# First products of a fused attention and expert kernel: products nobody reads at the start, one load on another queue, three-operand forms, and a regrouped end of the first expert's rows

## The chip, the cores and the metric

The kernel runs on one core of one Trainium2 chip, in one launch. The metric is the device time of that launch in microseconds (us), the median of three runs. The engines are TensorE (PE; its weight loads are shown apart as PEld), VectorE (DVE), ScalarE (ACT), GpSimd (POOL) and SyncE (SP), which here only issues DMAs.

## The reference, cut to what matters

```python
# attention: B=2, H=8, S=576, D=64; causal window of 128 keys, a linear bias per head
scores = where(mask, q @ k.T / 8 + bias[head], -1e9); attn = softmax(scores); x = attn @ v
x = x.transpose(0, 2, 1, 3).reshape(1152, 512)            # 1152 tokens, 512 wide
# experts: E=8, F=1024, capacity 288; each token goes to its best expert
logits = x @ w_gate; e = argmax(logits); gate = softmax(logits)[e]
disp[e, count[e]] = x[i]                                   # in order of the tokens, up to the capacity
y = relu(disp @ w1) @ w2; out[i] = gate[i] * y[e, pos[i]]
# then a dense layer, 512 -> 2048 -> 512, with h * sigmoid(h) between
```

## The kernel before

**Attention.** The 1152 tokens are 10 blocks (`NTOK`) of 128 rows; blocks 4 and 9 have 64. For each block t the loop at L1204 to L1241 gives PE this order: scores of the first four heads, the transposes of the probabilities, the turn of x of block t-2 with its logits, the values, the transpose of q of block t+1 (`turn(..., qraw)`), scores of the other four heads, transposes of their probabilities, the transpose of k of block t+1, and the values. DVE adds the bias and finds the minimum (L795), ACT takes the exponentials (L613) and copies q and k out of PSUM (`take_q`, `take_k`, L596 and L602). SP loads q, k and v of every block, in that order, by `load_qkv` (L330).

**Routing.** DVE finds each block's best expert (`first_match`), its places (`place_found`) and gate, and POOL multiplies x by the gate (L538) and scatters the rows to `dispatch_dram` (`scatter`, L518). For the last three blocks (t = 7, 8, 9, from `LAST`) ACT multiplies by the gate (`gate_x`, L675). The scattered rows of the seven blocks before them come back by one load (`load_first_slots(0)`, L362); PE brings them into the first expert's columns by products with the identity (L1270). The rows of the last three blocks do not wait for memory: POOL builds a 0/1 matrix of the slots (`select_first`, L524 to L529), and PE multiplies by it (`selected`, L1195), adding into the same four banks, `FIRST_X`. The turn of each bank c of the four is: two products with the identity, then the one product of block 9. ACT (L692) and DVE (L1008) take the bank as a high and a low part, `xT`.

**Experts.** PE goes through eight experts, most used first. Each is eight steps `up` of one F chunk, four steps `turn` that transpose the next expert's rows (`turn_slots`, L1284 to L1287), and four steps `down`. The first `turn` waits for `xd_in` and, because the second expert's width 200 is over `FIRST` = 192, for `xd_rest` too (L1326 to L1328). These come from SP, in this order (L399 to L415): it waits for the plan that DVE makes at L962 to L981 (`plan_ready`), loads the second expert's `w1` (four pieces of 512 KB), waits for the scatters of all blocks, loads the other slots of expert 0, waits for PE's `step_done`, loads the next expert's first slots, waits until the other slots of expert 0 have landed (L368), and loads the next expert's other slots. Behind them comes `w2`.

**Weights.** Every weight is split into a high part (a copy to fp32r, `w_hi`) and a low part (`w_lo`, the difference, written over the raw one). For the first expert there are eight pieces. POOL makes the high part of piece t in block t (`high_here`) and its low part in block t+1 (`low_here`), for `EARLY` = 6 pieces; ACT makes the last two high parts behind its last `gate_x` (L686 to L688).

## Time and profile before

| | us |
|---|---|
| median of 3 runs | 460.9 (460.63 to 463.35) |
| the profiled execution, its own time | 460.6 |
| its span, from the first to the last instruction | 458.8 |
| PE busy in the span | 439.1 (96%) |
| POOL busy | 240.3 (52%) |
| DVE busy | 229.1 (50%) |
| ACT busy | 221.0 (48%) |
| share of PE in the chain that ended last | 82% |

So 1.8 us of the launch lie outside the span, and the profiled execution is 0.3 us under the median. The page's slices show PE at 90% or more in nearly all of them. The granted clock of TensorE is given as a share of its full speed; the mean over the span is 0.991.

### The profile page before, as it was taken

To read this page: it belongs to the slowest core of one execution; us is meant where nothing else is said; L and a number is where in the kernel's file an instruction comes from. 1 tells how busy PE (TensorE), PEld (TensorE's weight loads), DVE (VectorE), ACT (ScalarE), POOL (GpSimd) and SP (SyncE) were. 2 spreads that over 40 slices of the span, in tenths; PEclk is the share of its full clock that TensorE was granted. 3 is DMA by queue.
4 is the path that set the end of the run, shared out by engine and by line. 5 is a ranking of instruction groups with operands and counts; after the bars stand their busy time and mean duration, and the time that the engine had idled before them with its cause. 6 is when DMAs were issued, how large, how long until landed. Compare 5 with 4: busy or idle time off the path is not lost.

```text
span 458.8 us, 8374 instructions
## 1 busy us (share of the span) xinstructions
PE 439.1 (96%) x2917; PEld 397.0 (87%) x2917; DVE 229.1 (50%) x732; ACT 221.0 (48%) x549; POOL 240.3 (52%) x172
## 2 busy tenths in 40 slices
PE   5999999899999999999999999999999999999993
PEld 4687778679999999999999999998999989999982
DVE  4478588878475775865854552222222231322230
ACT  4777778645576556656677643131212222221230
POOL 4005888856979989999999987502000002000002
PEclk9999999998999999999999999999999999999997
DMA  9999970038987767786887400001000001000002
GB/s 180 268 289 270 280 209 14 24 114 300 367 279 278 251 221 244 290 301 239 267 299 241 164 1 1 0 3 67 2 0 0 0 0 69 0 0 0 0 0 74
DMA packets 54568, 64.29 MB, mean 140 GB/s; under 512 B 32096, under 2 KB 32096, under 8 KB 54528
## 3 DMA queue, kind: packets, MB, share of 16 engines
q1 hardware_dynamic: 52752, 59.08, 41.6%
q0 software_dynamic: 1776, 4.73, 2.8%
q8 instruction: 20, 0.33, 0.3%
q14 instruction: 20, 0.16, 0.1%
HBM read 54.35 MB, written 9.44 MB: 139 GB/s over the span
## 4 chain that ended last, share of the span: by engine, by line
PE 82%; DVE 7%; ACT 7%; issue 2%; DMA 1%; POOL 1%; POOLq 0%; DVEq 0%
PE bank L1280 15%; PE bank L1281 14%; PE bank L1282 14%; PE bank L1302 14%; PE bank L1301 7%; PE bank L1121 4%; PE bank L1138 3%; DVE w_lo L1038 3%; PE bank L1299 3%; PE bank L1172 2%; PE bank L1160 2%; ACT prob L613 2%; PE bank L1105 2%; ACT w_hi L643 2%; PE bank L1300 1%
## 5 line engine op out<-in xcount | busy, mean ns | idle before, releaser
L490 POOL TENSOR_TENSOR w_lo<-w_raw,w_hi 128x1024 fp32r<-128x1024 f32 x72 | 179.2, 2520 | 16.1 <-ACT w_hi L643 14.5
L1072 DVE TENSOR_TENSOR g_full<-bank,sigmoid 128x384 f32<-128x384 f32 x48 | 26.8, 558 | 130.0 <-ACT sigmoid L730 124.8
L584 POOL DMA_INDIRECT out_dram<-out_stage,permcol x9 | 8.8, 973 | 150.8 <-ACT out_stage L750 147.5
L730 ACT ACTIVATE sigmoid<-bank 128x384 f32<-128x384 f32 x48 | 23.6, 492 | 125.4 <-PE bank L1282 116.6
L643 ACT ACTIVATE w_hi<-w_raw 128x1024 fp32r<-128x1024 f32 x74 | 77.8, 1053 | 0.0
L1003 DVE TENSOR_REDUCE bank<-bank 128x192 f32<-128x384 f32 (+5 forms) x96 | 49.0, 512 | 38.7 <-PE bank L1302 38.7
L1280 PE MATMUL bank<-x_hi,w_hi 128*128 x192 | 65.0, 338 | 0.0
L1282 PE MATMUL bank<-x_hi,w_lo 128*128 x192 | 64.6, 336 | 0.0
L1281 PE MATMUL bank<-x_lo,w_hi 128*128 x192 | 64.4, 336 | 0.0
L1302 PE MATMUL bank<-hidden,w_hi 128*128 128x384 f32 (+5 forms) x224 | 63.0, 351 | 0.0
L1280 PE MATMUL bank<-w_hi,g_hi 128*128 128x512 f32 x144 | 56.9, 395 | 0.8 <-DVE g_lo L1076 0.8
L1302 PE MATMUL bank<-xT,w_hi 128*128 128x384 f32 (+5 forms) x192 | 57.4, 354 | 0.0
L1281 PE MATMUL bank<-w_lo,g_hi 128*128 128x512 f32 x144 | 56.5, 392 | 0.0
L1301 PE MATMUL bank<-hidden,w_lo 128*128 128x192 f32 (+5 forms) x224 | 55.6, 248 | 0.7 <-DVE hidden L1018 0.6
L1282 PE MATMUL bank<-w_hi,g_lo 128*128 128x512 f32 x144 | 56.1, 389 | 0.0
L1301 PE MATMUL bank<-xT,w_lo 128*128 128x192 f32 (+5 forms) x192 | 48.8, 254 | 0.0
L613 ACT ACTIVATE prob<-prob,neg_max 128x256 f32<-128x256 f32 (+2 forms) x80 | 37.3, 469 | 19.8 <-DVE neg_max L795 19.7
L1301 PEld LDWEIGHTS bank<-hidden,w_lo 128*128 128x128 f32 x224 | 42.7, 190 | 2.0 <-DVE hidden L1018 1.9
L1302 PEld LDWEIGHTS bank<-hidden,w_hi 128*128 128x128 f32 x224 | 42.2, 188 | 0.0
L1280 PEld LDWEIGHTS bank<-x_hi,w_hi 128*128 128x128 f32 x192 | 36.1, 188 | 1.7 <-issue 0.2
L1281 PEld LDWEIGHTS bank<-x_lo,w_hi 128*128 128x128 f32 x192 | 36.0, 188 | 1.5
L1301 PEld LDWEIGHTS bank<-xT,w_lo 128*128 128x128 f32 x192 | 37.1, 193 | 0.0
(146 smaller groups left out, 792.1 us busy)
## 6 DMA issues: line engine op xcount, KB each, us to landing
w_raw<-in_moe_w_dram SPq DMA_DIRECT2D x64, 512.0 KB, 5.9
dispatch_dram<-zeros SPq DMA_DIRECT2D x4, 1152.0 KB, 8.0
w_raw<-in_moe_w_in_dram SPq DMA_DIRECT2D x8, 512.0 KB, 5.0
w_raw<-in_moe_w_out_dram SPq DMA_DIRECT2D x8, 512.0 KB, 6.1
dispatched<-dispatch_dram SPq DMA_DIRECT2D x9, 384.0 KB, 7.6
q_raw<-in_q_dram SPq DMA_DIRECT2D x8, 256.0 KB, 5.5
k_raw<-in_k_dram SPq DMA_DIRECT2D x8, 256.0 KB, 5.8
v_raw<-in_v_dram SPq DMA_DIRECT2D x8, 256.0 KB, 5.9
```

The source lines that it names most:

```text
L490: nc.gpsimd.tensor_tensor(wlo[s][:, sl], raw[s][:, sl], whi[s][:, sl], ALU.subtract).then_inc(pool_lo, 1)
L613: nc.scalar.activation(prob[0:r, u % 2, m, c0:c0 + n], prob[0:r, u % 2, m, c0:c0 + n], ACT.Exp, bias=nmin[0:r, t % 2, h:h + 1], scale=-1.0 ...
L643: nc.scalar.activation(whi[s][:, sl], raw[s][:, sl], ACT.Copy).then_inc(whi_ready, 1)
L730: nc.scalar.activation(sig[:, f % 2, :], bank[f % 4][:, 0:TB], ACT.Sigmoid).then_inc(sig_ready, 1)
L1003: nc.vector.tensor_reduce(bk[:, 0:w], both, axis=AX.X, op=ALU.add).then_inc(summed, 1)
L1072: nc.vector.tensor_tensor(gf[:, f % 2, :], bank[f % 4][:, 0:TB], sig[:, f % 2, :], ALU.mult).then_inc(gf_ready, 1)
L1121: last = nc.tensor.matmul(bS[u % 2][hh][0:r, j * 2 * P + c0:j * 2 * P + c0 + n], qT[d, t % 2, hp, 0:r], kT[d, hp, k0:k0 + n], start=True, ...
L1280: nc.tensor.matmul(dst, ah, bh, start=first, stop=False)
L1281: nc.tensor.matmul(dst, ah, bl, start=False, stop=False)
L1282: return nc.tensor.matmul(dst, al, bh, start=False, stop=last)
L1301: nc.tensor.matmul(dst, al, x[:, 0, 0:w], start=False, stop=False)
L1302: return nc.tensor.matmul(both, ah, x[:, :, 0:w], start=False, stop=last)
```

## The change

1. PE multiplies the identity by itself five times (`WAKE`) into a bank of the probabilities before its first transpose. Nobody reads the result.
2. The load of k of block 0 is issued by ACT, as its first instruction, and no longer by SP between q and v.
3. `EARLY` falls from 6 to 5: POOL makes one high part (in block 5) and one low part (in block 6) fewer, ACT makes three high parts instead of two, the first two of them earlier, behind `take_xT(9)` and behind `gate_exp(9)`, and POOL makes two low parts behind its last scatter instead of one.
4. `sums_guarded` (L813) and the one-hot of `first_match` (L868) become three-operand instructions with a tile of zeros as the third operand.
5. The slot matrix of block 9 is made by DVE behind `slot_found(9)` and ahead of the plan, not by POOL. POOL's three last scatters wait for `last_slots` instead. Two memsets at the start zero the rows that block 9 lacks, and `selected` takes 128 rows for it instead of 64.
6. PE brings the rows from memory into all four banks first, then multiplies block 9's rows into all four.

```diff
-    EARLY = 6
+    EARLY = 5
+    WAKE = 5
@@ SP, load_qkv
+                    if t == 0 and src is k:
+                        continue
@@ POOL
+            nc.gpsimd.memset(xg[:, NTOK - 1, :], 0.0)
+            nc.gpsimd.memset(sel[:, NTOK - 1 - LAST, :], 0.0)
...
-            for t in range(LAST, NTOK):
+            for t in range(LAST, NTOK - 1):
                 select_first(t)
             pool.wait_ge(xd_in, 16)
+            pool.wait_ge(last_slots, NTOK - LAST)
             for t in range(LAST, NTOK):
                 scatter(t)
             pool.wait_ge(plan_ready, 2)
-            low_here(1, EARLY - PIECES, EARLY + 1)
+            for n in range(EARLY, POOLED):
+                low_here(1, n - PIECES, n + 1)
@@ ACT
+            act.dma_start(kraw[0:ROWS[0], 0, :].rearrange("p (h d) -> p h d", h=H),
+                          k[0, :, 0:ROWS[0], :].rearrange("h p d -> p h d")).then_inc(k_in[0], 16)
...
             take_xT(NTOK - 1)
+            act.wait_ge(pool_lo, EARLY)
+            weight_high(1, EARLY - PIECES, 16)
             gate_x(NTOK - 2)
             gate_exp(NTOK - 1)
+            weight_high(1, EARLY + 1 - PIECES, 16)
             gate_x(NTOK - 1)
-            act.wait_ge(pool_lo, EARLY)
-            for p in range(EARLY, SPLITS):
+            for p in range(EARLY + 2, SPLITS):
                 weight_high(1, p - PIECES, 16)
@@ DVE
-                start(nc.vector.tensor_scalar_add(rsum1[0:r, :], rsum[0:r, t % 3, :], 1e-9))
+                start(nc.vector.scalar_tensor_tensor(rsum1[0:r, :], rsum[0:r, t % 3, :], 1e-9, zeros[0:r, 0:H], ALU.add, ALU.add))
...
-                nc.vector.tensor_scalar(onehot[0:r, t, :], wdesc[0:r, :], best[0:r, at_t], None, ALU.is_equal).then_inc(onehot_ready, 1)
+                nc.vector.scalar_tensor_tensor(onehot[0:r, t, :], wdesc[0:r, :], best[0:r, at_t], zeros[0:r, 0:E],
+                                               ALU.is_equal, ALU.add).then_inc(onehot_ready, 1)
...
             slot_found(NTOK - 1)
+            r = ROWS[-1]
+            dve.wait_ge(last_slots, NTOK - LAST)
+            nc.vector.tensor_scalar(sel[0:r, NTOK - 1 - LAST, :], slot_no[0:r, :], place[0:r, NTOK - 1:], sbase[0:r, NTOK - 1:],
+                                    ALU.subtract, ALU.is_equal).then_inc(last_sel, 1)
@@ PE
-                return nc.tensor.matmul(FIRST_X[c][:, 0:FIRST], xg[0:r, t, c * P:(c + 1) * P], sel[0:r, t - LAST, :],
+                return nc.tensor.matmul(FIRST_X[c][:, 0:FIRST], xg[:, t, c * P:(c + 1) * P], sel[:, t - LAST, :],
...
             pe.wait_ge(ident_ready, 1)
+            for _ in range(WAKE):
+                nc.tensor.matmul(bP[0][:, 0:P], ident[:], ident[:], start=True, stop=True)
...
-                if c == 0:
-                    pe.wait_ge(sel_ready, 3)
-                    pe.wait_ge(gated, NTOK)
+            pe.wait_ge(last_sel, 1)
+            pe.wait_ge(gated, NTOK)
+            for c in range(KC):
                 selected(NTOK - 1, c, False, True).then_inc(step_done, 1)
```

## Rows read from the trace of the kernel before

**Rows 1.** The timeline of PE in the first 22 us: start, duration, instructions, idle before.
```profile
4.20 1.09 PE L1105 MATMUL bank<-ident,q_raw 128*128 128x128 f32 x4 [4.20 <-DMA q_raw<-in_q_dram]
...
7.08 1.22 PE L1121 MATMUL bank<-kT,qT 64*128 64x128 f32 x8 [0.69 <-ACT kT L602]
...
13.09 2.08 PE L1121 MATMUL bank<-kT,qT 64*128 64x256 f32 x8 [0.69 <-ACT kT L602]
...
17.02 0.65 PE L1105 MATMUL bank<-ident,q_raw 128*128 128x128 f32 x4
17.60 1.13 PE L1121 MATMUL bank<-kT,qT 64*128 64x256 f32 x8
```

**Rows 2.** The timeline of all engines at the start: identity, k, ACT's exponentials.
```profile
1.24 0.29 POOL L458 TENSOR_SCALAR_AFFINE_SELECT ident<-ident 128x128 f32<-128x128 f32 x1 [0.24 <-POOL ident L461]
...
5.28 0.71 PEld L1105 LDWEIGHTS bank<-ident,k_raw 128*128 128x128 f32 x4 [0.39 <-DMA k_raw<-in_k_dram]
...
11.58 0.19 ACT L613 ACTIVATION_READ_ACCUMULATOR prob<-prob,neg_max 128x1 f32 x1
```

**Rows 3.** The chain that ended last, its first piece: start, duration, what.
```profile
0.79 3.27 DMA q_raw<-in_q_dram
```

**Rows 4.** DVE beside POOL late in the attention (timeline of both engines).
```profile
85.55 2.35 POOL L490 TENSOR_TENSOR w_lo<-w_raw,w_hi 128x1024 fp32r<-128x1024 f32 x1
...
87.18 0.76 DVE L813 TENSOR_SCALAR row_sum<-row_sum 128x8 f32<-128x8 f32 x1
```

**Rows 5.** Lines L813 and L868: duration ns min/median/max, first and last start.
```profile
L813 DVE TENSOR_SCALAR row_sum<-row_sum x10: 152/161/760, 22.8 to 92.9; 128x8 f32<-128x8 f32 x8, 64x8 f32<-64x8 f32 x2
...
L868 DVE TENSOR_SCALAR onehot<-wdesc,best x10: 223/231/306, 26.7 to 95.2; 128x8 fp32r<-128x8 f32 x8, 64x8 fp32r<-64x8 f32 x2
```

**Rows 6.** The timeline where the first expert's rows are built (all engines).
```profile
94.17 0.72 ACT L675 ACTIVATE x_gated<-x_tile,gate 128x512 f32<-128x512 f32 x1 [1.42 <-DVE gate L897]
...
96.11 1.55 PE L1198 MATMUL bank<-selection,x_gated 128*128 128x192 f32 x8
...
96.81 0.72 ACT L675 ACTIVATE x_gated<-x_tile,gate 64x512 f32<-64x512 f32 x1 [1.63 <-DVE gate L897]
...
97.27 0.15 DVE L965 TENSOR_SCALAR values<-bank 128x8 f32<-128x8 f32 x1
...
97.49 0.58 PE L1270 MATMUL bank<-ident,dispatched 96*128 96x96 f32 x4
98.50 0.59 PE L1198 MATMUL bank<-selection,x_gated 64*128 64x192 f32 x2 [0.43 <-POOL selection L528]
...
102.67 0.69 PE L1299 MATMUL bank<-xT,w_hi 128*128 128x384 f32 x1
```

**Rows 7.** DVE's bias instructions at the start (timeline): eight of 256 columns.
```profile
2.96 2.84 DVE L902 TENSOR_SCALAR bias<-rel 128x256 f32<-128x256 f32 x8 [2.96 <-POOL rel L458]
```

**Rows 8.** Windows of 1 us: length, busy of each engine, granted clock, DMA share, GB/s.
```profile
103.00:104.00 1.00, 1.00 (x5) 1.00 (x5) 0.36 (x1) 0.11 (x1) 1.00 (x1) 0.50 0.70 246
...
106.00:107.00 1.00, 1.00 (x9) 1.00 (x9) 0.83 (x6) 0.00 (x0) 0.00 (x0) 1.00 1.03 422
```

**Rows 9.** SP's issues in the timeline, behind the plan.
```profile
101.40 1.94 SPq L340 DMA_DIRECT2D w_raw<-in_moe_w_dram  x4
105.80 0.35 SPq L370 DMA_DIRECT2D dispatched<-dispatch_dram  x1
...
111.03 0.33 SPq L370 DMA_DIRECT2D dispatched<-dispatch_dram  x1
```

**Rows 10.** The tile view of `dispatched`: time to landing of L370's issues at 105.80 and 111.03.
```profile
DMA to landing us min/median/max: 5.1/5.1/5.1
...
DMA to landing us min/median/max: 2.4/2.4/2.4
```

**Rows 11.** The chain where `up` ends and `turn` begins: start, duration, what.
```profile
113.44 0.12 issue
113.56 1.18 PE bank L1286 x12
```

More of the change, by code:

```diff
@@ L211, in build @@
         gate_ready, gated, slot_ready, dve_step = sem("gate_ready"), sem("gated"), sem("slot_ready"), sem("dve_step")
-        last_slots, sel_ready = sem("last_slots"), sem("sel_ready")
+        last_slots, sel_ready, last_sel = sem("last_slots"), sem("sel_ready"), sem("last_sel")
         rest_turned, rest_high, rest_parts = sem("rest_turned"), sem("rest_high"), sem("rest_parts")
@@ L1195, in selected @@
             def selected(t, c, first, last):
-                r = ROWS[t]
-                return nc.tensor.matmul(FIRST_X[c][:, 0:FIRST], xg[0:r, t, c * P:(c + 1) * P], sel[0:r, t - LAST, :],
+                return nc.tensor.matmul(FIRST_X[c][:, 0:FIRST], xg[:, t, c * P:(c + 1) * P], sel[:, t - LAST, :],
                                         start=first, stop=last)
             pe.wait_ge(ident_ready, 1)
+            for _ in range(WAKE):
+                nc.tensor.matmul(bP[0][:, 0:P], ident[:], ident[:], start=True, stop=True)
             turn(0, qraw, q_in, bX)
```

## The prediction

> **What bounds the kernel now.** I read the page first: PE is busy for 96% of the span and holds 82% of the chain that ended last, so a change pays where it shortens PE's stream or a wait that PE ends up sitting in. From the slices and windows I took two stretches that the diff touches: the start, and the 95th to 115th us, where the attention hands over to the experts. In the timeline of PE at the start the reader should see that equal work takes different times: four transposes 1.09 us at 4.20 and 0.65 at 17.02, eight score products of 256 columns 2.08 at 13.09 and 1.13 at 17.60 [rows 1]. So PE ran at the lower of its clocks up to about 17 us, though the windows print a granted clock of 1.00 there (no change of clock is on record before it). The second such stretch is on record: 0.50 at 103 us (1.2 GHz), 1.00 again from 106 (2.4 GHz) [rows 8]. Third, the chain and SP's issues around 113 us: the first `turn` begins at 113.56, 0.12 us after the last `up` product gave way [rows 11], and the load it needs, issued at 111.03, took 2.4 us, to 113.43 [rows 9, 10]. The waits view names a DVE instruction for PE's stop of 0.3 us there, but that one had long been done; `turn` waits for three semaphores, and only the load fits. PE's stream and this load therefore end within 0.2 us of each other. That decides most of what follows.
>
> **The five products at the start.** The identity is ready at about 1.55 and q lands at 4.06 [rows 2, 3]. One 128-column transpose is 0.27 us at the low clock; a full fp32 product of the same columns is issued as two such records, as the scores are, so it costs at most 0.55 us and, by start to start, about 0.43. Five make 2.2 us (2.7 at worst) from 1.6: done at 3.8, or 4.3 at worst, so they cost 0 to 0.2 us. They do no work; what they can buy is the clock. If PE is at the high clock from the first scores at 7.08, those end 0.6 us earlier (half of 1.22), and so do the exponentials behind them. Then ACT is next: it was free of its exponentials at 11.77 [rows 2] and then waited for PE's transposes of k; 0.6 earlier that is 11.2, with 0.6 for the copy of k the scores of block 1 start at 11.8 instead of 13.09: 1.3 us. From there to the scores at 17.60 PE has 4.5 us of work at the low clock that take about 2.7 at the high one (2.08 to 1.1, and transposes, values and transposes of q at 0.6, 0.5 and 0.6): another 1.8. Together 3.1 us, and everything behind it moves with it, because the attention is one chain of PE, DVE and ACT, and the loads of w1, w2 and the plan follow that chain. Low end 0 (the clock does not come earlier), high end 3.5 (it is high for the first transposes too).
>
> Does the clock rise? In the trace it stayed low through three us of transposes and 128-column scores from 7.08 on, with one gap of 0.7, and rose only after 13.09 to 17, when PE had no gap and long scores [rows 1]. With the five products PE is at work from 1.6 to 6.4 with one gap of under 1 us, which it never was there. I take it as somewhat likelier than not. The Trainium skill (TensorE: Matmul & The Clock Gate, Part 4: PE-mode transpose) says that transposes do not count as PE activity for the clock; the trace is in line with it, as the rise followed the scores, but it cannot part it from the gaps. By that rule the five products would be the first work that counts, and the sum would be the 3.1 to 3.5 us; with transposes counting alike it would be nearer 0 to 3.
>
> **k on ACT's queue.** k moves ahead by one issue and then shares the DMA engines with q. Before, q landed at 4.06 and PE's weight load waited 0.39 us for k until 5.28 [rows 2, 3]. Both together should be there by 4.7: q's transposes start up to 0.6 later, k's no longer wait. At the low clock that is a loss of up to 0.6 (4.7 + 2.2 = 6.9 against 6.4), at the high clock a gain of 0.4 (4.7 + 1.3 = 6.0). If the queues do not disturb each other, it is 0. I take 0, as the forecast's clock lies between the two. ACT's issue is hidden: it has nothing to do before the copy of q. The Trainium skill (DMA: Bandwidth & Descriptors, Issuing engines are not separate DMA queues) speaks against a gain: such loads interleave on the same engines, and only the issuer's time is saved. By it the sum would carry the +0.6 where the clock stays low.
>
> **The three-operand forms.** Ten of each. L813 has a median of 161 ns and L868, with a rounded output, 231 [rows 5]; the nearest three-operand times lie between, so each may cost 0 to 0.08 us. Only those of the blocks where DVE ends the chain count, about four of twenty: 0 to +0.3. What they may save: L813 took 0.76 us at 87.18, until POOL's low part of 85.55 ended [rows 4], one more was long. The work behind both waits for ACT's copy of x anyway, which ended later, so the 0.6 us hide. Value +0.1, bounds −0.3 to +0.3.
>
> **POOL's and ACT's pieces.** POOL loses a high part (1.06) and the low part at 85.55 (2.35) in the attention; scatter 6 leaves 1.5 us earlier, but PE took its rows at 97.49 straight behind block 8's products (96.11 and 1.55), so it did not wait for them [rows 6]. ACT's added high parts take 1.05 us each and go into its idle 1.42 and 1.63 us ahead of `gate_x` [rows 6]; behind them wait the two `gate_x` and PE's products. That cover is thin: if `gate` comes earlier by more than 0.4, ACT ends it. POOL's second late low part (2.4 us) ends near 106, and the first `down` asks behind `turn`, at 114.7 [rows 11]. All 0.
>
> **The regrouped rows.** Before, from 97.49 to 102.67, 5.2 us [rows 6]: 0.43 waiting for POOL's matrix, then product and selection in turn. After: four product groups of 0.58 and four selections that with 128 rows take 1.55 together, as block 8's did: 3.9 us, ready at 101.4. Gain 1.2 us at PE. With it PE is denser, so that the low clock of 102 to 105.5, which costs half of 3.4, may not come: another 1.7. `up` would end 1.2 or 2.9 us earlier than 113.44.
>
> **But the first `turn` waits for the load.** Its chain is plan, w1 (101.40), the other slots of expert 0 (105.80, 5.1 us behind the 2 MB of w1), then the next expert's (111.03, 2.4) [rows 9, 10]. Nothing PE gains enters it. What does: DVE's matrix for block 9 stands ahead of the plan. The bias instructions cost 0.35 each for 256 columns [rows 7]; 192 columns and the wait for `slot_i` give 0.4 (0.3 to 0.5; never the 1.0 of POOL). Queued behind: the plan, excess, SP's w1 and so the load. Against it, POOL's scatters start 1.1 us earlier and leave the DMA engines to w1 sooner, worth 0 to 0.5. Net +0.2 (−0.2 to +0.5). So the 1.2 to 2.9 us become idle time of PE ahead of `turn`.
>
> **Sum.** Profiled span 458.8: start −3.1 taken at −2.7, as the clock may come a little later than the first scores, k 0, forms +0.1, regrouping 0, plan +0.2: 456.4. With the 1.8 us outside the span and 0.3 from the profiled time to the median: 458.5.
>
> **The rivals.**
> A, the forecast, 0.45: start pays, handover is swallowed: 458.5, own range 457.4 to 459.8.
> B, 0.30, ends slower: the clock does not rise before the 13th us. Then only the costs are left: k +0.6, forms +0.1, plan +0.2, and 461.8. The point from which it decides: the four transposes at about 5 us and the scores at 13 us keep 1.09 and 2.08. For it: the record of 7 to 12 us above.
> C, 0.13: the load isn't the bound, because w1 with no scatter beside it lands over 1 us earlier; then 1.2 to 2.9 of the handover count: with the middle, 2.0, 456.5 with A, 459.8 with B. Against it: four pieces of w1 already ran back to back.
> D, 0.07: the clock falls behind 106 instead, since PE idles ahead of `turn`; 1.7 us at PE are lost where nothing hides them: 460.2 with A, 463.5 with B.
> E, 0.05: the change does nothing: 460.9.
>
> **Range and chances.** The ends are C at its full 2.9 with A, rounded down for a high start (455.3), and B with the upper bounds of plan and forms (+0.5 more: 462.3); B with D and the corners left out hold about 0.1. Within 1% is 456.3 to 465.5, about what a measurement can tell from no change. Faster than that needs C with A and most of its gain: 0.1. Slower needs B, D and more: 0.03.
>
> **What would show it.** A: transposes near 0.6 us at 5 to 8 us, the scores of block 1 at about 11.5 to 12, the first `up` near 98.7 (101.5 minus the shift), and an idle PE of 1 to 3 us ahead of the first L1286. B: long scores at 13 us. C: no such idle time, L1286 over 5 us earlier than 113.56. D: a granted clock of 0.50 behind 110. My forecast fails if PE doesn't wait ahead of `turn`, or if the first 17 us keep their length.

## The result and the profile after

| | before | after |
|---|---|---|
| median of 17 runs each, us | 461.9 (460.63 to 471.70) | 464.4 (461.98 to 476.46) |
| ratio of the times, 95% interval | | 1.0048 [1.0028, 1.0068] |
| profiled execution, its own time, us | 460.6 | 467.3 |
| its span, us | 458.8 | 465.6 |
| its mean granted clock | 0.991 | 0.977 |
| first product of the first expert, us | 102.67 | 104.72 |
| first `turn`, us | 113.56 | 117.83 |
| first `up` product of the second expert, us | 123.78 | 130.55 |
| first product of the dense layer, us | 249.87 | 256.88 |

Ratios and means here and below leave out the executions more than 1.5% above the fastest of the same kernel; medians are over all. The changed kernel is 0.5% slower, 464.4 us where 458.5 was forecast and 462.3 was the upper end. Before itself came out 1.0 us higher in 17 runs than in the three shown ahead; against the three alone, 460.9, the ratio makes 463.1, still above the range. The profiled execution of after is one of its longer ones (467.3 with a median of 464.4) and ran at the lowest mean clock of them (0.977; the mean of the 14 is 0.988), so the places of its losses count here, not their sum.

The timeline of PE in the changed kernel, first 22 us, to be laid beside [rows 1]:

```profile
1.57 2.50 PE L1218 MATMUL bank<-ident 128*128 128x128 f32 x10 [1.57 <-POOL ident L461]
4.62 1.11 PE L1121 MATMUL bank<-ident,q_raw 128*128 128x128 f32 x4 [0.54 <-DMA q_raw<-in_q_dram]
5.53 1.06 PE L1121 MATMUL bank<-ident,k_raw 128*128 128x128 f32 x4
7.27 1.22 PE L1137 MATMUL bank<-kT,qT 64*128 64x128 f32 x8 [0.69 <-ACT kT L609]
...
13.28 2.08 PE L1137 MATMUL bank<-kT,qT 64*128 64x256 f32 x8 [0.69 <-ACT kT L609]
...
17.38 0.66 PE L1121 MATMUL bank<-ident,q_raw 128*128 128x128 f32 x4
17.97 1.13 PE L1137 MATMUL bank<-kT,qT 64*128 64x256 f32 x8
```

The five products (ten records) fill 1.57 to 4.07, and the clock takes no notice: transposes 1.11 us, block 1's scores 2.08, the short forms only from 17.38. q's transposes start at 4.62 for 4.20, k's no longer wait, the first scores start at 7.27 for 7.08. That is rival B's sign.

The windows of the changed kernel at the handover (stretch in us, its length, then busy time and instructions of PE, PEld, DVE, ACT, POOL; granted clock, DMA share, GB/s):

```profile
106.00:111.00 5.00, 5.00 (x37) 5.00 (x36) 4.79 (x8) 0.00 (x0) 3.52 (x2) 1.00 0.99 395
111.00:114.00 3.00, 3.00 (x22) 2.87 (x20) 2.86 (x10) 1.53 (x4) 0.17 (x1) 1.00 0.92 236
114.00:115.00 1.00, 0.12 (x1) 0.00 (x0) 1.00 (x3) 1.00 (x2) 1.00 (x1) 1.00 0.06 18
115.00:116.00 1.00, 0.00 (x0) 0.00 (x0) 1.00 (x4) 0.47 (x2) 1.00 (x1) 1.00 0.04 14
116.00:117.00 1.00, 0.00 (x0) 0.00 (x0) 1.00 (x4) 0.71 (x2) 1.00 (x2) 0.66 0.85 211
117.00:120.00 3.00, 2.17 (x13) 2.20 (x14) 2.53 (x8) 2.98 (x8) 3.00 (x2) 0.50 0.93 315
120.00:123.00 3.00, 3.00 (x12) 3.00 (x12) 0.54 (x2) 0.36 (x2) 3.00 (x2) 0.50 1.02 377
123.00:126.00 3.00, 3.00 (x22) 3.00 (x22) 0.83 (x2) 1.28 (x2) 1.06 (x2) 0.97 1.03 417
```

PE is busy without a break to 114.1, then idle to 117.83, and in that idle time, at about 116.3, the granted clock falls to 0.50 (1.2 GHz), where it stays until 123.2. From 120 to 123 PE is fully busy and gets through 12 instructions, from 123 to 126 through 22. Before had its short low stretch ahead of this, from 102.1 to 105.5 [rows 8], and none behind it before the last microseconds of the span. The same profiled execution also ran at 0.50 from 89.0 to 99.3, 10.2 us where before had 3.4; with it the first expert starts 2.05 us later although the regrouped rows took less.

The chain that ended last in the changed kernel, between 103 and 120 us (start, duration, what), and SP's DMA issues there (start, duration of the issue):

```profile
103.82 3.60 DMA dispatch_dram<-x_gated,slot_i
...
107.44 7.66 DMA dispatched<-dispatch_dram
...
115.25 2.45 DMA dispatched<-dispatch_dram
117.70 0.14 issue
117.83 2.15 PE bank L1303 x12
```
```profile
104.37 1.93 SPq L343 DMA_DIRECT2D w_raw<-in_moe_w_dram  x4
107.44 0.35 SPq L373 DMA_DIRECT2D dispatched<-dispatch_dram  x1
108.06 0.34 SPq L365 DMA_DIRECT2D dispatched<-dispatch_dram  x1
115.25 0.33 SPq L373 DMA_DIRECT2D dispatched<-dispatch_dram  x1
```

It is the chain of [rows 9 to 11] with two differences. All of it is 3.0 us later here (w1 at 104.37 for 101.40). And the other slots of expert 0 took 7.7 us to land instead of 5.1 [rows 10], so the load that the first `turn` waits for went out 10.9 us behind w1, not 9.6.

### The profile page after: what moved, and what is told of

It reads as the page before. It is cut to its first block, busy times and chain, and to the rows that moved or that the text cites. A ratio compares the mean times of both kernels' runs of the same rounds, so it can differ in the third digit from the quotient of the medians.

```text
span 465.6 us, 8394 instructions
## 1 busy us (share of the span) xinstructions
PE 445.0 (96%) x2927; PEld 404.0 (87%) x2927; DVE 230.4 (49%) x733; ACT 222.0 (48%) x550; POOL 238.8 (51%) x172
## 4 chain that ended last, share of the span: by engine, by line
PE 77%; ACT 8%; DVE 8%; DMA 4%; issue 2%; POOL 0%; POOLq 0%; SPq 0%
PE bank L1297 14%; PE bank L1298 14%; PE bank L1299 14%; PE bank L1319 12%; PE bank L1318 6%; PE bank L1137 4%; DVE w_lo L1054 3%; PE bank L1154 3%; PE bank L1176 3%; PE bank L1188 2%; ACT prob L620 2%; DMA dispatched<-dispatch_dram 2%; ACT w_hi L650 2%; PE bank L1316 2%; PE bank L1121 2%
## 5 line engine op out<-in xcount | busy, mean ns | idle before, releaser
L650 ACT ACTIVATE w_hi<-w_raw 128x1024 fp32r<-128x1024 f32 x75 | 78.9, 1053 | 0.0
L1319 PE MATMUL bank<-hidden,w_hi 128*128 128x384 f32 (+5 forms) x224 | 64.3, 356 | 0.0
```

The lines of the kernel that those rows point to most:

```text
L650: nc.scalar.activation(whi[s][:, sl], raw[s][:, sl], ACT.Copy).then_inc(whi_ready, 1)
L1319: return nc.tensor.matmul(both, ah, x[:, :, 0:w], start=False, stop=last)
```

## The experiments

Each kernel ran with runs of before on the same chip; before had medians of 461.4 to 462.7 us in the sessions, and single runs behind its means from 459.2 to 465.9 us. "Ratio" is that of the times to before's, with its 95% interval. "Mean" is the kernel's mean time, beside 461.8 to 462.2 for before; "clock" is its mean granted clock, 0.989 to 0.991 for before.

| kernel | median us | ratio [95%] | mean us | clock |
|---|---|---|---|---|
| p_start | 461.6 | 1.0003 [0.9976, 1.0031] | 461.8 | 0.990 |
| p_early | 462.0 | 1.0019 [0.9989, 1.0049] | 462.5 | 0.988 |
| p_forms | 461.7 | 1.0006 [0.9977, 1.0035] | 462.1 | 0.988 |
| p_rows | 465.8 | 1.0095 [1.0061, 1.0129] | 465.8 | 0.982 |
| x_rows_order | 462.8 | 0.9990 [0.9956, 1.0024] | 462.7 | 0.991 |
| x_rows_keep | 462.6 | 0.9986 [0.9956, 1.0015] | 462.3 | 0.994 |
| x_after_order | 462.3 | 1.0000 [0.9976, 1.0025] | 462.4 | 0.993 |
| x_before_order | 462.5 | 0.9977 [0.9948, 1.0006] | 461.7 | 0.990 |
| x_after_keep | 463.1 | 1.0016 [0.9987, 1.0044] | 462.6 | 0.994 |
| x_after_order2 | 464.8 | 1.0051 [1.0021, 1.0080] | 464.2 | 0.988 |
| x_before_order2 | 464.6 | 1.0060 [1.0030, 1.0091] | 464.7 | 0.986 |
| x_wake12 | 463.9 | 1.0040 [1.0015, 1.0066] | 463.7 | 0.986 |
| x_after_skip | 464.2 | 1.0034 [1.0002, 1.0065] | 463.7 | 0.990 |
| x_wake12_split | 464.0 | 1.0034 [1.0011, 1.0058] | 463.7 | 0.985 |
| x_before_split | 463.3 | 1.0029 [1.0014, 1.0044] | 463.3 | 0.984 |
| x_after_skip_split | 463.2 | 0.9999 [0.9965, 1.0033] | 462.1 | 0.990 |
| x_after_skip_keep | 461.8 | 1.0006 [0.9981, 1.0031] | 462.1 | 0.994 |

### One part at a time

**p_start**: before with parts 1 and 2 only.

```diff
+                    if t == 0 and src is k:
+                        continue
@@ ACT, first instruction
+            act.dma_start(kraw[0:ROWS[0], 0, :] ...)
@@ PE
+            for _ in range(WAKE):
+                nc.tensor.matmul(bP[0][:, 0:P], ident[:], ident[:], start=True, stop=True)
```

> Only the start of the change: five unread products and block 0's k on ACT's queue. Theory H (the loss is made in the handover, by the first expert's rows): +0.3 us, the shift of the first scores from 7.08 to 7.27 that the changed kernel shows, and no more. Rival S (the start makes the loss: it costs more in other executions than in the profiled one, or shifts the blocks so that the clock falls at a worse place): +1.5 to +3 us. If the clock came up earlier in some executions, this kernel would be faster by up to 3 us.

**p_early**: part 3 only (`EARLY = 5`, ACT's two high parts moved ahead of its last `gate_x`, POOL's second late low part).

> Only EARLY = 5: one high and one low part fewer on POOL in the attention, ACT's high parts in the gaps ahead of gate_x. Theory H: 0 +- 0.5 us. Rival E (ACT's high part of 1.05 us delays gate_x, and through it PE's products and the scatter; or POOL is now the one that is late behind the last scatter): +1 to +2.5 us.

**p_forms**: part 4 only, the two three-operand forms.

> Only the three-operand forms of L813 and L868. Theory H: 0 to +0.3 us. A rival in which they wait for POOL's low parts longer than the old forms did: +1 us or more, with L813 or L868 near 0.7 us in several blocks.

**p_rows**: parts 5 and 6 only, block 9's matrix on DVE and the regrouped products.

> Only the first expert's rows: block 9's matrix by DVE ahead of the plan, 128 rows, PE takes all rows from memory first. Theory H: +1.5 to +2.5 us, nearly the whole loss; excess 0.5 us or more later behind slot_i, PE idle for 2 us or more ahead of the first turn (0.12 before), and in some executions a granted clock of 0.50 behind 110 us. Rivals S and E: 0 +- 0.5 us.

Parts 1 to 4 cannot be told from nothing. Parts 5 and 6 alone lose 3.7 us (1.0095, seven runs), more than the 1.5 to 2.5 expected and more than the full change. Their profile has the wait and the low clock, with no other part of the change in it. The line of `turn` in PE's timeline of p_rows, then its windows:

```profile
114.20 2.15 PE L1292 MATMUL bank<-ident,dispatched 96*128 96x96 f32 x12 [3.55 <-DMA dispatched<-dispatch_dram]
```
```profile
112.00:115.00 3.00, 0.80 (x5) 0.83 (x6) 1.35 (x4) 1.38 (x4) 3.00 (x2) 0.79 0.69 204
115.00:118.00 3.00, 3.00 (x17) 3.00 (x15) 1.10 (x3) 1.30 (x4) 3.00 (x2) 0.50 0.98 356
118.00:121.00 3.00, 3.00 (x15) 3.00 (x14) 0.29 (x1) 0.00 (x0) 0.07 (x1) 0.58 1.05 409
121.00:124.00 3.00, 3.00 (x23) 3.00 (x22) 1.36 (x4) 1.56 (x4) 1.24 (x1) 1.00 1.03 419
```

The rows are ready early (the first `up` at 101.25, before at 102.67), as forecast. PE then idles 3.55 us, the clock is at 0.50 from 113.7 to 120.5, `turn` comes 0.6 us later than before's, the second expert 13.2 us behind `turn` where before had 10.2. 0.6 and 3.0 make 3.6; the two profiled spans differ by 3.3 (462.1 and 458.8), the means by 3.7.

### Is it the wait, the clock, or something else?

**x_rows_order**: p_rows, with the other slots of expert 0 and both loads of the next expert's slots between the halves of w1.

```diff
-            load_w1(expert[1], 2)
+            load_w1(expert[1], 2, range(2))
             ...
+            load_w1(expert[1], 2, range(2, PIECES))
```

> p_rows with another order of SP's issues: only two pieces of the second expert's w1 ahead of the loads of the slots, the other two behind them. Theory I (the loss is PE's idle time ahead of the first turn, which waits for xd_rest behind 2 MB of w1, and the clock that falls after it): the first turn begins 2 us or more earlier than 114.2, PE is idle for under 1 us ahead of it, no granted clock of 0.50 follows, and the time is 4 to 6 us under p_rows, 0.5 to 2.5 under before. Rival J (the clock falls because of the sparse products of the whole handover, whatever the first turn waits for): the fall behind the first turn stays and the gain over p_rows is 0 to 2 us.

**x_rows_keep**: p_rows, with 14 products of the identity ahead of the first `turn`, into the bank that `turn` overwrites; nobody reads them.

```diff
+                        if c == 0 and e == 0:
+                            for _ in range(14):
+                                nc.tensor.matmul(bk[:, 0:P], ident[:], ident[:], start=True, stop=True)
```

> p_rows with 14 unread products of the identity by itself (0.22 us each at the high clock, some 3 us) ahead of the first turn. The wait for xd_rest stays as it is; only PE isn't idle in it. Theory I, its second half (the idle time makes the clock fall, and that costs more than the wait): no fall behind 110 us, first turn at about 114.2 as in p_rows, second up near 124.5 instead of 127.4, the time 2.5 to 3.5 us under p_rows and 0.5 to 1.5 over before. If the clock falls all the same, 0 to 1 us under p_rows.

**x_after_order**, **x_before_order**: the first edit on after and on before.

> The changed kernel with the same order of SP's issues as x_rows_order. Theory I: its loss of 2.5 us goes and 1 to 2 us of gain come in its place, so 0.5 to 2 us under before. Rival J: it stays at +1 to +2.5 us.

> The kernel before with the same order of SP's issues alone. PE waited 0.12 us there, so Theory I: 0 to -0.5 us. If the order is worth something by itself (w1 or w2 arriving at a better time), or costs something (w1's last pieces late for ACT), it shows here: beyond -1 or +1 us.

Both cures take the loss away: 462.7 and 462.3 for 465.8, clear of noise against p_rows. Neither brings the gain over before (0.5 to 2.5 us) that x_rows_order was expected to show. The second leaves the transfers as they are and only keeps PE at work; it raises the mean clock from 0.982 to 0.994, and 3.4 of the 3.7 us come back. So most of p_rows' price is the low clock behind the wait, not the wait. (The one profile of x_rows_keep has a span of 601 us, so only its times are used.) In x_rows_order `turn` starts at 113.80 without waiting and no low stretch follows; but the second half of w1 goes out only at 110.84, and PE then waits for it: the second expert's `up` comes at 126.28, later than before's 123.78. This order of loads has a price of its own there.

**x_after_keep**: after, with the same 14 products.

> The changed kernel with 14 unread products of the identity ahead of the first turn. If the loss of the changed kernel is what the idle time ahead of the first turn does to the clock: no granted clock of 0.50 begins within 7 us behind 110 us, the second expert's first up comes 10 us behind the first turn (12.7 in the changed kernel, 10.2 in the one before), and the time is 1.5 to 2.5 us under the changed kernel, within 0.5 us of before. If that was peculiar to p_rows: no difference to the changed kernel, +2.5 us over before.

**x_after_order2**, **x_before_order2**: as the order edit, but the second half of w1 ahead of the next expert's other slots.

```diff
-            load_w1(expert[1], 2)
+            load_w1(expert[1], 2, range(2))
             ...
-            load_dispatched(expert[1])
+            load_first_slots(expert[1])
+            load_w1(expert[1], 2, range(2, PIECES))
+            load_other_slots(expert[1])
```

> The changed kernel with w1's last two pieces issued behind the second expert's first slots and ahead of its other slots, so that they don't wait for a landing (in x_after_order they were issued at 111 us, and the down steps and the second up came late). If the handover's gain of about 1.2 us at PE is real and was only given back to loads: first turn at about 112, second up 10 us behind it, 1 to 2 us under before. If the order of the loads is not what holds it: no difference to x_after_order, 0 to +0.5 us over before.

> The kernel before with the same order of loads as x_after_order2, alone. It waited 0.12 us ahead of the first turn: 0 to -0.5 us. A gain beyond -1 us would say that executions other than the profiled one wait there for longer.

x_after_keep, PE's timeline and two of its windows:

```profile
111.24 3.29 PE L1344 MATMUL bank<-ident 128*128 128x128 f32 x28
115.27 1.18 PE L1303 MATMUL bank<-ident,dispatched 96*128 96x96 f32 x12 [0.75 <-DMA dispatched<-dispatch_dram]
```
```profile
112.00:115.00 3.00, 2.52 (x23) 2.33 (x21) 2.98 (x9) 2.17 (x5) 3.00 (x2) 1.00 0.28 85
115.00:118.00 3.00, 2.73 (x24) 2.76 (x25) 2.36 (x7) 2.54 (x8) 3.00 (x2) 1.00 0.93 317
```

The chain of loads still takes its time (the last one issued at 112.60, `turn` at 115.27), but the idle piece of PE ahead of it is 0.75 us and the clock stays at 1.00; `turn` takes 1.18 us, not 2.15, and the second expert comes 10.2 us behind it, as in before. The mean is 462.6 us, for 464.4 of the full change; the ratios, 1.0016 [0.9987, 1.0044] and 1.0048 [1.0028, 1.0068], overlap at their edges, so on the full change the cure is less certain in the times than on p_rows.

x_before_order2 was expected to change nothing (0 to −0.5 us) and missed, and so became a test from the other side: a kernel with none of the change's parts, in which one load was put behind 1 MB of w1. Its line of `turn` and its windows:

```profile
116.00 2.15 PE L1288 MATMUL bank<-ident,dispatched 96*128 96x96 f32 x12 [3.06 <-DMA dispatched<-dispatch_dram]
```
```profile
115.00:118.00 3.00, 2.00 (x13) 2.03 (x14) 1.09 (x3) 2.23 (x5) 3.00 (x3) 0.50 1.05 371
118.00:121.00 3.00, 3.00 (x13) 3.00 (x13) 0.37 (x1) 0.38 (x2) 1.86 (x1) 0.50 1.05 402
```

With the wait of 3.06 us comes the low clock (114.8 to 121.6), the second expert 12.9 us behind `turn` instead of 10.2, and 464.6 us, 1.0060 [1.0030, 1.0091]. x_after_order2 missed too, 464.8 us where up to 2 us under before were hoped for: PE waited 2.20 us, `turn` came at 116.31, and here the clock fell only 1.0 us into the work, at 117.3, until 120.7. The first edit, without the piece of w1 ahead of the load, cured after (x_after_order: `turn` at 113.42, 462.3 us) and moved before by less than can be told from nothing.

**x_after_skip**: after, where SP leaves out the other slots of expert 0 when nobody is in them (`excess` is 0 here).

```diff
-            load_other_slots(0)
+            n_over = sp.value_load(excess[0:1, 0:1], min_val=0, max_val=C)
+            with sp.If(n_over <= 0):
+                sp.sem_inc(xd_rest, 16)
+            with sp.Else():
+                load_other_slots(0)
+            loaded[0] = 1
```

> The changed kernel; SP leaves out the load of expert 0's other slots where all widths suffice (nobody reads them then), so that the second expert's other slots are issued some 4 us earlier, behind w1 and its first slots. Theory I: the first turn waits no longer for a landing that waits for a landing; it begins about 112, PE is idle under 1.5 us ahead of it, the clock doesn't fall there, and the time is 2 to 4 us under the changed kernel, 0 to 1.5 us under before. Rival: other loads land late instead and it stays over before by 1 us or more.

Its own profile, PE's line of `turn`, SP's issues, and a window:

```profile
113.91 1.18 PE L1308 MATMUL bank<-ident,dispatched 96*128 96x96 f32 x12 [2.76 <-DMA dispatched<-dispatch_dram]
```
```profile
101.75 1.87 SPq L343 DMA_DIRECT2D w_raw<-in_moe_w_dram  x4
105.54 0.33 SPq L365 DMA_DIRECT2D dispatched<-dispatch_dram  x1
106.09 0.35 SPq L373 DMA_DIRECT2D dispatched<-dispatch_dram  x1
```
```profile
115.00:118.00 3.00, 3.00 (x24) 3.00 (x23) 2.62 (x9) 2.29 (x7) 3.00 (x2) 1.00 1.06 399
```

One load less in the chain, and the load that `turn` needs goes out at 106.09, 5 us earlier than before's; yet it lands 7.7 us later, at 113.8, 12.0 us behind the 2 MB of w1 issued at 101.75, as in before (12.0; 13.3 in after). That fits w1's bytes setting when the loads behind them arrive, not their number; no run changed the bytes alone. PE's wait is still 2.76 us, where under 1.5 was expected. This execution kept its clock and took 460.9 us. The eleven runs behind the mean fall apart: four took 460.9 to 462.3 us at 0.990 to 0.995, two 463.4 and 463.8 at 0.992, five 464.6 to 467.1 at 0.984 to 0.987. The likeliest reading is that after a wait near 3 us the clock sometimes falls and sometimes does not; only one execution has a trace.

**x_after_skip_keep**: x_after_skip, with 14 unread products. The expectation places them ahead of the first `turn`; the edit placed them elsewhere, ahead of the first `up` product of the first expert.

```diff
                     if kind == "up":
                         if c == 0:
                             pe.wait_ge(pool_lo, pooled_by(e, PIECES))
+                        if c == 0 and e == 0:
+                            for _ in range(14):
+                                nc.tensor.matmul(bk[:, 0:P], ident[:], ident[:], start=True, stop=True)
```

> The changed kernel with both remedies at the first turn: SP leaves out the other slots of expert 0 when nobody is in them, and 14 products whose results are not read keep PE at work ahead of the turn. If the idle time ahead of the turn and the low clock behind it are the whole of what the changed kernel loses, this one should keep a mean clock near 0.993, show no granted clock of 0.50 behind 110 us, and take 461.0 to 462.0 us, 1 to 2 us less than skipping alone (463.7). If they are not the whole, it stays at 462.4 to 463.7, as the unread products alone did (462.6).

PE's timeline shows where they ran:

```profile
101.89 3.36 PE L1344 MATMUL bank<-ident 128*128 128x128 f32 x28 [0.85 <-issue]
114.27 1.16 PE L1308 MATMUL bank<-ident,dispatched 96*128 96x96 f32 x12
```

So this run does not fill the wait; it sends PE there 3 us later. The first `up` comes at 105.01, `turn` at 114.27 without a wait (its load had landed at 114.0), no low clock behind 110: 461.8 us, mean 462.1, 0.994, level with before, though PE carries 3.1 us of useless work. That bears out that PE's time ahead of `turn` is bounded by the load. The interval (0.9981 to 1.0031) overlaps that of x_after_skip (1.0002 to 1.0065), so the difference of 1.6 us between the two means is not clear of noise.

### Does an earlier clock at the start pay?

**x_wake12**: p_start with `WAKE = 12`.

> p_start with twelve unread products instead of five: they run from 1.6 to about 6.7 us, so q's transposes begin some 2.2 us later than the load allows. Theory F (five are too few, a longer stretch without a gap lifts the clock): the clock is at 1.0 by 8.5 us, the transposes of q of block 1 take near 0.6 us, and the gain of 3 us pays for the delay: -1.5 to +0.5 us. Theory G (unread products of this kind do not lift it, only the later stretch does): the clock rises at 11 to 17 us as before and the time is +1.5 to +2.5 us.

Twelve products do lift the clock, but the time does not come down to the range that was expected in that case (−1.5 to +0.5 us): the mean is 1.6 over before's. PE's timeline at the start:

```profile
1.58 4.72 PE L1208 MATMUL bank<-ident 128*128 128x128 f32 x24 [1.58 <-POOL ident L461]
6.14 0.60 PE L1110 MATMUL bank<-ident,q_raw 128*128 128x128 f32 x4
```

Transposes take 0.60 us from 6.14, block 1's scores start at 12.66 for 13.09 and take 1.13 for 2.08. The exponentials lead before's by 2.1 us at 21 us (21.05 for 23.16) and still at 44 (44.24 for 46.38). Then, all engines between 54 and 57 us:

```profile
54.17 2.35 POOL L493 TENSOR_TENSOR w_lo<-w_raw,w_hi 128x1024 fp32r<-128x1024 f32 x1
54.27 2.28 DVE L818 TENSOR_SCALAR row_sum<-row_sum 64x8 f32<-64x8 f32 x1
```

A DVE operation on 8 columns takes 2.28 us, until POOL's low part of 54.17 ends. Its median in before is 161 ns [rows 5]. At 62 us the lead has become a lag of 1.2 (62.29 for 61.07). The same row took 2.02 us in p_start and 2.17 in x_rows_order, whose clocks rose at 10.9 and 11.3 us. In before, whose clock rose at 16.8, two were hit, by 0.58 and 0.76 only [rows 4, 5]. The Trainium skill (SBUF — State Buffer, Who interferes with whom) says that DVE and GpSimd share a pair of ports, and that where an instruction of DVE takes that pair, whoever issues first has it for a whole instruction and the other is blocked. The trace agrees: DVE's row starts 0.10 us behind POOL's and ends at 56.55, POOL's at 56.52.

**x_wake12_split**, **x_before_split**: x_wake12 and before, each low part of the attention cut into four operations of 256 columns. **x_after_skip_split**: x_after_skip with the same cut.

```diff
-                nc.gpsimd.tensor_tensor(wlo[s][:, sl], raw[s][:, sl], whi[s][:, sl], ALU.subtract).then_inc(pool_lo, 1)
+                for n in range(cuts):
+                    w = PIECE // cuts
+                    sl = slice(part * PIECE + n * w, part * PIECE + (n + 1) * w)
+                    last = nc.gpsimd.tensor_tensor(wlo[s][:, sl], raw[s][:, sl], whi[s][:, sl], ALU.subtract)
+                last.then_inc(pool_lo, 1)
@@ the blocks of the attention
-                    low_here((t - 1) // PIECES, (t - 1) % PIECES, t)
+                    low_here((t - 1) // PIECES, (t - 1) % PIECES, t, 4)
```

> x_wake12 with POOL's low parts of the attention cut into four instructions of 256 columns. Theory K (a short DVE instruction that meets a running low part waits for its end): no L813 or L868 over 0.8 us, the blocks keep their 2 us ahead of before, and the time is 1.5 to 3 us under x_wake12. Rival L (the early gain is lost to another engine or load that paces the blocks): the short instructions are short and the time stays within 0.7 us of x_wake12.

> The kernel before with the low parts of the attention cut in the same way, alone. Theory K: executions of before that were hit by such a stall gain up to 2 us, those that were not gain nothing, so -0.3 to -1.5 us in the median and a narrower spread. Rival L: 0, or +0.5 us for the added instructions on POOL.

> The changed kernel with both, the load left out and the low parts cut. If both theories hold, it beats before by 1 to 3 us; if only I holds, it is equal to x_after_skip.

At this place the mechanism holds. The timeline of x_wake12_split:

```profile
54.22 2.78 POOL L495 TENSOR_TENSOR w_lo<-w_raw,w_hi 128x256 fp32r<-128x256 f32 x4
54.77 0.19 DVE L821 TENSOR_SCALAR row_sum<-row_sum 64x8 f32<-64x8 f32 x1
```

The stalled row is back at 0.19 us, the four parts take POOL 2.78 us instead of 2.35, and the lead lives on to 75.08 us (before 76.15, x_wake12 77.44). One row further on, at 86.12, still took 1.11 us, over the 0.8 expected at most. The time does not follow: mean 463.7 with and without the cut. What goes right in the attention is gone at the handover: both executions have 6.8 us at 0.50 there (from 94.1 and from 92.9), and `turn` at 116.10 and 116.07, where before has 113.56. In before, where a gain of 0.3 to 1.5 us was expected, the cut costs: 463.3 us at 0.984, 1.0029 [1.0014, 1.0044]. Its profile has a low clock from 46.9 to 53.7, in the middle of the attention, and again around 95 and 105 us. That POOL's longer parts cause this was not tried.

In x_after_skip_split the mean is 462.1 us, level with before (0.9999 [0.9965, 1.0033]) and 1.6 under x_after_skip, not clear of noise. The gain of 1 to 3 us over before that it was expected to show if both theories hold did not come. Its profile shows where a real lead goes: `turn` at 111.11, the second expert at 122.37 for 123.78, the dense layer at 248.78 for 249.87. Then, from the timelines of DVE and PE:

```profile
254.39 2.84 DVE L1100 TENSOR_TENSOR g_lo<-g_full,g_hi 128x384 fp32r<-128x384 f32 x1
257.46 0.50 PE L1305 MATMUL bank<-w_hi,g_hi 128*128 128x512 f32 x1 [2.00 <-DVE g_lo L1100]
```

The median of this DVE operation is 548 ns; here it ran beside POOL's low parts, which follow each other from 249.71 to 262.16, and PE waited 2.00 us for it. The span is 459.8 us, for before's 458.8.

## Why the prediction was wrong

**The start, −2.7: nothing measured (p_start: 1.0003 [0.9976, 1.0031]), and a false link.** The arithmetic of the products was right (2.50 us against 2.2 worked out and 2.7 at worst, nothing lost by them) and so was the direction in which a fast clock moves the block (x_wake12 was 2.1 us ahead at 21 us; p_start and p_rows, with the clock up only at about 11, were as far ahead). Two steps failed. First, "I take it as somewhat likelier than not" that five products lift the clock. It rested on a misreading: that PE at work from 1.6 to 6.4 with one gap of under 1 us is something "which it never was there". Between the rows at 7.08 and 13.09 of [rows 1], PE's timeline of before goes on:

```profile
8.23 1.11 PE L1105 MATMUL bank<-ident,q_raw 128*128 128x128 f32 x4
9.28 1.23 PE L1121 MATMUL bank<-kT,qT 64*128 64x128 f32 x8
10.43 1.11 PE L1138 MATMUL bank<-ident,prob 128*128 128x128 f32 x4
11.34 1.06 PE L1105 MATMUL bank<-ident,k_raw 128*128 128x128 f32 x4
```

So PE was at work there from 4.20 to 12.40, 8.2 us with one gap of 0.69, longer than the stretch that the five products would give, and the clock stayed low. The products do not lift it: with them it rose at 17.3 (after), 10.9 (p_start), 13.1 (x_after_order), 11.2, 11.4, 17.1, 11.2 and 10.8 us; in executions without them at 16.8 (before), 17.2, 16.4, 11.3, 11.3, 11.8, 12.4 and 12.8. (These are read from the lengths of like products; 13.1, 12.4 and 12.8 fall in an idle time of PE from about 12.5 to 13.2 and are no better than that.) That is the same spread, and before's 16.8 was one draw from it, not the kernel's property. The sum took its gain against a row that five of those eight do not have. By the rule on transposes that the prediction cites from the Trainium skill, the five products should have brought 3.1 to 3.5; no run with five shows that. The same page (TensorE: Matmul & The Clock Gate, Part 1) says that the number of slow products at the start differs from run to run of one kernel, and these traces agree (one each of kernels that are alike in these microseconds). Second, "everything behind it moves with it". It does not: the lead ends in DVE waiting for POOL at 54 us, or at the handover. The start won with twelve products (x_wake12) went with a kernel 0.4% slower, and spans do not follow the rise: 458.8 us with the rise at 16.8 (before), 459.5 at 17.2 (x_before_order), 459.2 at 17.1 (x_after_skip), 458.9 at 10.9 (p_start), 460.2 at 11.8 (p_early).

**k on ACT's queue, 0.** With the clock low, the forecast said a loss of up to 0.6; the first scores came 0.19 later in after and 0.28 in p_start, without an effect that the times show.

**The forms, +0.1.** p_forms: 1.0006 [0.9977, 1.0035]; the row took 148 to 160 ns in after for 161, the one-hot 219 to 227 for 231. Right. The form does not keep out of POOL's way either: in p_forms the three-operand row still took 752 ns once.

**POOL's and ACT's pieces, 0.** p_early: 1.0019 [0.9989, 1.0049]. Right within what it can tell.

**The regrouped rows, 1.2 us.** In after, 3.75 us from 100.97 to the first `up` at 104.72, for 5.18 us: 1.4. Right.

**"So the 1.2 to 2.9 us become idle time of PE ahead of `turn`."** Right in kind, and this is where the forecast broke. It priced the idle time at nothing, since the load was the bound. In the runs the idle time is what costs: 3.5 to 3.7 us without work, then 6.8 us at 1.2 GHz, which end the next 10.2 us of work 3.0 us later (p_rows; 2.5 in after). Rival D named this mechanism but was given 0.07 and 1.7 us, the price of before's shorter low stretch; "463.5 with B" was within 1 us of the result. What was missing is the question what an idle PE does to the work behind it, put to the forecast's own case and not to a corner. Before's 0.12 us of wait ahead of `turn` [rows 11] was itself one draw: its low stretch of 3.4 us fell into the `up` steps and used the wait up. In kernels without parts 5 and 6, where the low stretch came ahead of the steps, PE waited 0.77 us (p_forms), 0.82 (x_wake12) and 2.00 (p_early), and the clock held. Likewise the 1.7 us that the forecast hoped for from a low stretch that stays away are a draw, not a gain of the regrouping: in p_rows it came at 93.2.

**The plan, +0.2.** `excess`, the plan's last row, came 2.86 us behind `slot_i` of block 9 in before, 3.13 in after and 3.14 in p_rows: +0.3, as priced. SP did not pass it on: w1 went out 1.40 us behind `excess` in before, 1.13 in both others. So the load's chain began no later, counted from `slot_i`.

**The landing, not foreseen.** The term "Net +0.2 (−0.2 to +0.5)" stands for the load's chain. It measured +1.2. The other slots of expert 0 took 5.1 us to land in before, 7.6 in p_rows, 7.7 in after. There they were issued 3.1 us behind w1, in before 4.4; counted from w1's issue the load landed after 9.5 and 10.7 us. x_after_keep has 10.5, and of the kernels without parts 5 and 6 p_forms, p_early and x_wake12 have 9.5 to 9.8, though x_before_split has 10.4. 1.2 us later at the load that `turn` needs is what made the idle time of p_rows 3.6 us long, longer than the 1.2 to 2.9 forecast. Why it lands later although it is issued earlier stays open; the scatters end ahead of it in both.

**How much of the whole change's loss is the clock.** An estimate: a microsecond at 0.50 while PE works costs half a microsecond, so a mean clock lower by 0.01 costs at most 4.6 us of 460. For p_rows (0.982 for 0.989) that is 3.2 of 3.7 us. For the full change (0.988 for about 0.990, before's in the sessions of the table) it is only about 1 of 2.5 us, and six of its fourteen runs have 0.991 to 0.994 and still a mean of 463.4. So the low clock behind the wait explains p_rows and the profiled execution of after, but on average only part of what the full change loses; the late landing of 1.2 us is there at a full clock too (x_after_keep: `turn` at 115.27, a span of 460.6). The rest stays open. So does why the whole change loses less than its parts 5 and 6 (464.4 and 465.8); the intervals of the two ratios, 1.0028 to 1.0068 and 1.0061 to 1.0129, overlap, so it may be no difference.

In short: the step that failed first is the earlier clock at the start, priced at −2.7 and worth nothing. The step that turned no gain into a loss is the idle time ahead of `turn`, priced at 0: it was 3.6 us long for 1.2 to 2.9, because the load landed 1.2 us later, and in p_rows it cost 3.0 us more through the clock.

## What to carry to other kernels

Before shortening PE's work ahead of a load that it already meets within a fraction of a microsecond, work out what PE does in the time gained: in p_rows 3.6 us without work cost 3 us more behind it through the clock, and products that nobody reads took that price away again. A level of the clock, its moment of rising, or a wait of 0.12 us, read from one profile is one draw: look at it in several executions before it enters a sum. And a stage that starts earlier meets its neighbours at other moments; ask which engine it will collide with (here DVE with POOL's low parts of 2.35 us and more, in the attention and again in the dense layer) before adding its gain to the end.

## What the runs showed of the hardware

- The granted clock fell during an idle time of PE of 3.1 to 3.7 us that followed several us of full work, and then stayed at 0.50 for 6.8 us although PE was at work again: after, p_rows, x_before_order2. In x_after_skip a wait of 2.8 us left it at 1.00, in p_early one of 2.0, and with the 14 products ahead of it (x_after_keep) one of 0.75. In x_after_order2 it fell 1.0 us into the work behind a wait of 2.2, for 3.4 us. So no length of wait read here divides the two.
- Kernels alike in their first microseconds, with and without five unread products, saw the clock rise anywhere from 10.8 to 17.3 us. Between 89 and 108 us all but two of the profiles (x_after_skip, x_after_skip_keep; x_rows_keep's not counted) show a low stretch of 3.4, 6.8 or 10.2 us, x_before_split two of 3.4, at a different place.
- With twelve unread products the clock was up by 6.14 us in x_wake12 and rose between 6.9 and 7.8 in x_wake12_split.
- A DVE operation on 8 columns took up to 2.28 us beside POOL's subtraction of two fp32 tiles (2.35 us), in both the one-tile and the two-tile form (x_after_order: 1.99 us for the three-operand row). Cut in four, POOL's operation took 18% longer and the longest of these rows 1.11 us. A DVE subtraction of two 128x384 tiles took 2.84 us for 0.55 beside POOL's run of the same (x_after_skip_split).
- 192 KB of slots issued 2.7 to 4.6 us behind 2 MB of w1 took 5.1 to 7.8 us to land (before, p_forms, p_early, x_before_split, p_rows, after, x_after_keep), and with the load between left out the next one, issued 4.3 to 4.6 us behind w1, landed 10.8 to 12.3 us behind it (x_after_skip_split, x_after_skip, x_after_skip_keep), with it 12.0 in before and 13.3 in after.
